# Attention groups from 20 on scored in pairs at new ticks, sums and roots turned by transposes, and fillers moved in the early ticks of a fused attention and expert kernel

## The reference, cut to what matters

```python
scores = (q @ k.T) / 8                        # 4 batches, 8 heads, 576 x 576, head dim 64
# heads 0-3: key within the last 32 positions; heads 4-7: key at a distance that is a multiple of 32
attn = softmax(where(mask, scores, -1e9)) @ v
x = attn as (2304, 512)
rms = sqrt(mean(x * x) + 1e-6)                # per token
xn = x / rms * rms_g
x = (silu(xn @ w_gate) * (xn @ w_val)) @ w_out      # 512 -> 1536 -> 512
logits = x @ router + modality_bias[modality_id]    # 8 experts, the best one is taken
out = softmax gate of that expert * (relu(x @ w1[e]) @ w2[e])   # 512 -> 1024 -> 512
```

## Time and profile before

| what | us |
|---|---|
| median of 3 runs (range) | 863.51 (862.11 to 865.79) |
| the profiled execution, its own time | 865.16 |
| its span in the trace | 863.4 |
| TensorE busy | 847.0 |
| VectorE busy | 535.7 |
| ScalarE busy | 369.6 |
| GpSimd busy | 330.5 |

### The profile page before, as it was taken

One profiled execution on the slowest core, in us unless ns is written; L12 is line 12 of the kernel. 1 busy time (PEld: TensorE's weight loads), 2 busy tenths in 40 slices (PEclk: granted clock), 3 DMA queues, 4 the chain that ended last, 5 costly groups with the idle time before them and its releaser, 6 DMA issues.

```text
span 863.4 us, 15547 instructions
## 1 busy us (share of the span) xinstructions
PE 847.0 (98%) x5203; PEld 732.6 (85%) x5203; DVE 535.7 (62%) x1400; ACT 369.6 (43%) x934; POOL 330.5 (38%) x373
## 2 busy tenths in 40 slices
PE   9999999999999999999999999999999999999996
PEld 5678898999889998999999998987888888888885
DVE  6975565444563446548788764884887457666663
ACT  6966414445354355443221132243456235554441
POOL 3735772434432633544346333070043122222212
PEclk9989999999999999999999999999999999999999
DMA  8974212312132210242131121626275645555531
GB/s 193 283 176 125 60 45 65 96 57 80 51 101 61 65 38 25 74 159 74 37 98 61 61 74 37 226 67 257 98 239 186 232 146 194 200 202 193 194 118 40
DMA packets 77517, 103.40 MB, mean 120 GB/s; under 512 B 38973, under 2 KB 43069, under 8 KB 77312
## 3 DMA queue, kind: packets, MB, share of 16 engines
q1 hardware_dynamic: 73760, 91.16, 33.5%
q0 software_dynamic: 3680, 11.28, 3.8%
HBM read 92.98 MB, written 10.22 MB: 120 GB/s over the span
## 4 chain that ended last, share of the span: by engine, by line
PE 86%; DVE 7%; issue 3%; POOL 2%; ACT 1%; DVEq 0%; POOLq 0%; ACTq 0%
PE ps L1251 31%; PE ps L1290 15%; PE ps L1855 13%; PE ps L1840 13%; PE ps L1176 3%; PE ps L1211 2%; PE ps L1865 2%; PE ps L1190 2%; PE ps L1150 2%; PE ps L1332 1%; PE ps L670 1%; DVE h L1641 1%; POOL sm L1046 1%; DVE h_lo L1646 1%; DVE w_lo L2094 1%
## 5 line engine op out<-in xcount | busy, mean ns | idle before, releaser
L1046 POOL TENSOR_TENSOR sm<-sm,rinv 72x288 f32<-72x288 f32 (+1 forms) x51 | 45.6, 893 | 168.8 <-DVE rinv L1577 168.8
L1078 POOL TENSOR_TENSOR out_lo<-out_raw,out_hi 128x512 fp32r<-128x512 f32 x72 | 101.8, 1414 | 5.8
L1076 POOL CAST out_hi<-out_raw 128x512 fp32r<-128x512 f32 x72 | 52.6, 730 | 132.9 <-DMA out_raw<-in_moe_w_out 132.9
L1251 PE MATMUL ps<-x_hi,gate_hi 128*128 128x384 f32 x288 | 100.1, 348 | 0.6 <-DVE h L1635 0.6
L1635 DVE SCALAR_TENSOR_TENSOR h<-h,ps 128x384 f32<-128x384 f32 x72 | 39.8, 552 | 97.4 <-ACT h L1469 96.5
L1251 PE MATMUL ps<-x_hi,val_hi 128*128 128x384 f32 x288 | 98.5, 342 | 0.0
L1251 PE MATMUL ps<-x_hi,gate_lo 128*128 128x384 f32 x288 | 96.9, 337 | 0.0
L1251 PE MATMUL ps<-x_hi,val_lo 128*128 128x384 f32 x288 | 96.4, 335 | 0.0
L1251 PE MATMUL ps<-x_lo,val_hi 128*128 128x384 f32 x288 | 96.3, 334 | 0.0
L1251 PE MATMUL ps<-x_lo,gate_hi 128*128 128x384 f32 x288 | 93.7, 335 | 0.0
L1290 PE MATMUL ps<-out_hi,h_hi 128*128 128x512 f32 x216 | 88.4, 409 | 1.3 <-DVE h_lo L1646 1.3
(11 more groups left out here) (288 smaller groups left out, 1937.8 us busy)
## 6 DMA issues: line engine op xcount, KB each, us to landing
w_raw<-in_moe_w SPq DMA_DIRECT2D x72, 512.0 KB, 4.4
out_raw<-in_moe_w_out SPq DMA_DIRECT2D x72, 256.0 KB, 2.6
x_rows<-y_tiles SPq DMA_DIRECT2D x18, 256.0 KB, 2.8
early_w_raw<-in_moe_w SPq DMA_DIRECT2D x8, 512.0 KB, 4.3
gate_raw<-in_moe_w_gate SPq DMA_DIRECT2D x4, 768.0 KB, 8.3
val_raw<-in_moe_w_val SPq DMA_DIRECT2D x4, 768.0 KB, 10.0
qk<-in_q SPq DMA_DIRECT2D x8, 288.0 KB
qk<-in_k SPq DMA_DIRECT2D x8, 288.0 KB
```

The source lines that it names most:

```text
L1046: pool.tensor_tensor(s3, s3, rinv[0:n, i, :].unsqueeze(2).to_broadcast([n, 4, c]), ALU.mult).then_inc(s_no, 1)
L1076: pool.tensor_copy(oh[i][:, :], o_raw[i][:, :]).then_inc(s_oh, 1)
L1078: pool.tensor_tensor(ol[i][:, :], o_raw[i][:, :], oh[i][:, :].bitcast(f32), ALU.subtract).then_inc(s_ol, 1)
L1251: mm = pe.matmul(ps[:, bank, 0:CH], w[:, i, kk, cols], x[:, kk, :], start=(m == 0), stop=(m == n - 1))
```

## The change

It changes places and distances of attention groups, the buffers, two small steps of the normalisation, and fillers.

- `PAIRS` is 20: groups 20 to 27 go in pairs, scored at ticks 22, 28, 40 and 52, turned at 32, 38, 50 and 62, multiplied at 34, 40, 52 and 64.
- The pairs from 28 on stand 4 ticks sooner: scored at 82, 94, ..., 238, which is (c, f, 1, 0) with f even, turned at (c, f, 0, 0), multiplied with the next pair's scores.
- `PLACE` uses four buffers throughout. Batch 1's second local head pair transposes q and k at ticks 34, 34, 36, 36 instead of 27, 29, 30, 32, in banks 6 and 5 by turns.
- For chunks 1 to 5 the sums over partitions are made by three transposes of the summed squares into bank 7, and VectorE reduces the 128 x 384 result. For all chunks the roots are spread by three transposes of the root column, broadcast along 128 columns; the tile of diagonals is gone.
- `square` waits only for the groups that hold tokens of its chunk. ScalarE's wait for the low parts of x at a batch's first pair now names batches 2 and 3, the only ones whose first group is in a pair before and after.
- Two fillers more at tick 16 between its scores and its turned probabilities, two more at tick 17 behind the sums, and two instead of three at the end of tick 17.

```diff
--- before.py
+++ after.py
@@ -61,8 +61,8 @@
     if j < HEAD:
         return j
     if j < 2 * NG:
-        return EARLY + 2 + 3 * (j - HEAD)
-    return EARLY + SPAN - 6 + 12 * ((j - 2 * NG) // 2)
+        return EARLY + (2, 8, 20, 32)[(j - HEAD) // 2]
+    return EARLY + SPAN - 10 + 12 * ((j - 2 * NG) // 2)
 
 
 def by_tick(ticks):
@@ -73,12 +73,12 @@
 
 
 SCORE = {j: score_tick(j) for j in range(G)}
-PAIRS = 2 * NG
+PAIRS = HEAD
 TURN = {j: SCORE[j] + (3 if j < HEAD - 3 else 7 if j < PAIRS else 10) for j in range(G)}
 TURN.update({HEAD - 3 + i: EARLY + 1 + 2 * i for i in range(3)})
 PV = {j: TURN[j] + (1 if j < HEAD - 1 else 2) for j in range(G)}
 
-PLACE = {j: j % SM if j < HEAD else (j - HEAD) % (SM - 1) for j in range(G)}
+PLACE = {j: j % SM for j in range(G)}
 PRIOR = {j: max((i for i in range(j) if PLACE[i] == PLACE[j]), default=None) for j in range(G)}
 
 EXPS = {j: SCORE[j] + (0 if j < HEAD - 1 else 1) for j in range(G)}
@@ -95,7 +95,9 @@
         return [0, 0, 0, 0]
     if s < EARLY:
         return {4: [1, 2, 2, 3], 8: [4, 5, 6, 7], 10: [7, 8, 8, 9], 14: [12, 12, 13, 13], 18: [14, 14, 15, 16]}[s]
-    return [s - 7, s - 5, s - 4, s - 2] if b < 2 else [s - 9, s - 9, s - 6, s - 6]
+    if b < 2:
+        return [s - 7, s - 5, s - 4, s - 2] if hp == 0 else [s - 6, s - 6, s - 4, s - 4]
+    return [s - 9, s - 9, s - 6, s - 6]
 
 
 QK = {(b, hp, t): qk_ticks(b, hp)[t] for b in range(B) for hp in range(4) for t in range(4)}
@@ -256,8 +258,8 @@
         sm_early = res.put("sm_early", [P, 512])
         sq_at = res.at
         sq = res.put("sq", [P, CH])
-        diag = alias("diagonals", sq_at, [P, TT, P])
         nr = res.put("squares_sum", [P, CH])
+        total = res.put("squares_total", [P, TT])
         var = res.put("variance", [P, TT])
         halved = res.put("halved_bits", [P, TT], i32)
         root = res.put("root", [P, TT])
@@ -442,8 +444,8 @@
         s_sq = sem("squares_steps")
         s_ssq = sem("squares_summed")
         s_nv = sem("variance_read")
+        s_va = sem("variance_made")
         s_nw = sem("newton_steps")
-        s_dg = sem("diagonals_made")
         s_rb = sem("roots_spread")
         s_rc = sem("roots_copied")
         s_xn = sem("normed_x")
@@ -519,7 +521,7 @@
 
         def qk_bank(b, hp, t):
             if QK[b, hp, t] >= FIRST_DOWN:
-                return 6 if b < 2 else 6 - t % 2
+                return 6 - t % 2
             if QK[b, hp, t] >= EARLY:
                 return 3 + QK_NO[b, hp, t] % 2
             return 4 if QK_NO[b, hp, t] % 2 else 0
@@ -1048,7 +1050,7 @@
 
             def square(c, kk):
 
-                first = max(i for i, (hp, g) in enumerate(GROUPS) if hp == kk and not (c == 0 and hp < 2 and g == 2))
+                first = max(i for i, (hp, g) in enumerate(GROUPS) if hp == kk and (hp > 1 or 2 * LQ * g <= (CH * c + CH - 1) % S))
                 pool.wait_ge(s_oe, NG * last_batch(c) + first + 1)
                 if c and kk == ORDER[0]:
                     pool.wait_ge(s_xn, KT * c)
@@ -1134,7 +1136,7 @@
                     per_load = 64 if is_loc(hp) else 32
                     pe.wait_ge(s_qk[hp], per_load * (b + 1))
                 if s >= FIRST_DOWN:
-                    pe.wait_ge(s_qe, no if b < 2 else no - t % 2)
+                    pe.wait_ge(s_qe, no - t % 2)
                     scores_read(s)
                     pe.wait_ge(s_pe, TURNED_PROBS[s])
                 elif TURNED_QK[QK_BY_ACT] == no:
@@ -1158,8 +1160,8 @@
                     pe.wait_ge(s_qe, QK_NO[b, hp, 3] + 1)
                 if j:
                     pe.wait_ge(s_m, 4 * (j if j < PAIRS else j - j % 2))
-                if j >= PAIRS:
-                    pe.wait_ge(s_pe, j - j % 2)
+                if TURNED_PROBS[s] > PAIRS:
+                    pe.wait_ge(s_pe, TURNED_PROBS[s])
                 if s >= FIRST_DOWN:
                     pe.wait_ge(s_qe, TURNED_QK[s])
                 for i in range(4):
@@ -1222,8 +1224,10 @@
                 pe.wait_ge(s_sq, sq_steps(c + 1))
                 for t in range(TT):
                     cols = slice(t * P, (t + 1) * P)
-                    mm = pe.matmul(ps[:, ss_bank(c), t:t + 1], nr[:, cols], ones[:, 0:1], start=True, stop=c > 0)
-                    if c == 0:
+                    if c:
+                        mm = pe.transpose(ps[:, ss_bank(c), cols], nr[:, cols], ident[:, :])
+                    else:
+                        pe.matmul(ps[:, ss_bank(c), t:t + 1], nr[:, cols], ones[:, 0:1], start=True, stop=False)
                         mm = pe.matmul(ps[:, ss_bank(c), t:t + 1], sq[:, cols], ones[:, 0:1], start=False, stop=True)
                 mm.then_inc(s_ssq, 1)
 
@@ -1231,9 +1235,11 @@
 
                 if c:
                     bank_7_free(("rb", c))
-                pe.wait_ge(s_dg, c + 1)
-                pe.matmul(ps[:, rb_bank(c), 0:CH], ones[:, :], diag[:, :, :].rearrange("p t n -> p (t n)"),
-                          start=True, stop=True).then_inc(s_rb, 1)
+                pe.wait_ge(s_nw, 11 * c + 11)
+                for t in range(TT):
+                    mm = pe.transpose(ps[:, rb_bank(c), t * P:(t + 1) * P], root[:, t:t + 1].to_broadcast([P, P]),
+                                      ident[:, :])
+                mm.then_inc(s_rb, 1)
 
             def product(bank, wh, wl, f, half, done, new=None):
 
@@ -1348,8 +1354,11 @@
                     keep_busy(2)
                 for j in SCORE_AT.get(s, []):
                     score(j)
+                if s == SS[0]:
+                    keep_busy(2)
                 if s == SS[0] + 1:
                     sum_squares(0)
+                    keep_busy(2)
                 for j in TURN_AT.get(s, []):
                     turn_probs(j)
                 for j in PV_AT.get(s, []):
@@ -1358,7 +1367,7 @@
                     for key in QK_AT.get(s, []):
                         turn_qk(*key)
                 if s < EARLY:
-                    keep_busy({16: 3, 17: 3, EARLY - 1: 4}.get(s, 2))
+                    keep_busy({16: 3, EARLY - 1: 4}.get(s, 2))
                 for c in SS_AT.get(s, []):
                     if c:
                         sum_squares(c)
@@ -1431,7 +1440,7 @@
                 b, hp, g = place(j)
                 n = rows(hp)
                 act.wait_ge(s_pv, j + 2)
-                if j % NG == 0:
+                if b >= 2 and j % NG == 0:
                     act.wait_ge(s_xl, KT * b)
                 src = ps[:, 7, :].rearrange("d (a x) -> d a x", a=2)[:, :, 0:2 * n]
                 if not is_loc(hp):
@@ -1594,10 +1603,18 @@
                     dve.wait_ge(s_nw, n_steps[0])
 
                 if c:
-                    dve.wait_ge(s_dg, c)
+                    dve.wait_ge(s_rb, c)
                 dve.wait_ge(s_ssq, c + 1)
-                dve.tensor_scalar(var[:, :], ps[:, ss_bank(c), 0:TT], 1.0 / DM, 1e-6, ALU.mult, ALU.add).then_inc(s_nv, 1)
-                dve.wait_ge(s_nv, c + 1)
+                if c:
+                    dve.tensor_reduce(total[:, :], ps[:, ss_bank(c), 0:CH].rearrange("p (t d) -> p t d", t=TT),
+                                      axis=AX, op=ALU.add).then_inc(s_nv, 1)
+                    dve.wait_ge(s_nv, c + 1)
+                    dve.tensor_scalar(var[:, :], total[:, :], 1.0 / DM, 1e-6, ALU.mult, ALU.add).then_inc(s_va, 1)
+                    dve.wait_ge(s_va, c)
+                else:
+                    dve.tensor_scalar(var[:, :], ps[:, ss_bank(c), 0:TT], 1.0 / DM, 1e-6,
+                                      ALU.mult, ALU.add).then_inc(s_nv, 1)
+                    dve.wait_ge(s_nv, 1)
                 link(dve.tensor_scalar(halved[:, :], var[:, :].bitcast(i32), 1, None, ALU.logical_shift_right))
                 link(dve.tensor_scalar(root[:, :].bitcast(i32), halved[:, :], -1.0, 1597463007.0, ALU.mult, ALU.add))
                 for i in range(3):
@@ -1606,9 +1623,6 @@
                     link(dve.tensor_tensor(newt[:, :], newt[:, :], var[:, :], ALU.mult))
                     link(dve.scalar_tensor_tensor(out=root[:, :], in0=newt[:, :], scalar=1.5, in1=root[:, :],
                                                   op0=ALU.add, op1=ALU.mult))
-                dve.wait_ge(s_sq, sq_steps(c + 1))
-                dve.tensor_tensor(diag[:, :, :], ident[:, :].unsqueeze(1).to_broadcast([P, TT, P]),
-                                  root[:, :].unsqueeze(2).to_broadcast([P, TT, P]), ALU.mult).then_inc(s_dg, 1)
 
             def normalise_x(c, kk):
 
```

## The result

The changed kernel takes 852.86 us (median of 4 runs, 851.78 to 853.54) against 862.86 for the kernel before measured beside it. The ratio is 0.987, interval 0.9846 to 0.9893. So 10 us were won where 13.1 were forecast; the time lies 2.5 us above the forecast 850.4 and inside its range. The profiled execution took 853.54, its span is 851.8.

A forecast was written before the change was run, and what follows sets the result against it. TensorE, busy 98% of the span, was taken as the bound. Terms 2.9 + 2.7 + 4.7 + 2.8 = 13.1 us off the median 863.5 gave 850.4, range 846.8 to 857.

The forecast's parts named there:

- A, the early ticks: Early ticks: fillers hold the clock up, root spread by three transposes; 2.9 us, or 0.2 if the clock falls.
- If they hold the clock up, the 6.8 us shrink: Early ticks, from about 47.3 us: fillers keep TensorE off the low clock, and that stretch gives back 3.0 us.
- the clock falls all the same: Rival for the early ticks: fillers do not stop the fall, gain there 0.2 instead of 2.9, time 853.1; chance 0.17.
- The margin of VectorE's path: Behind chunk 0's roots, before its first product at about 52.7: some 0.4 us to spare, so no cost.
- B, pairs from 20: Singles 20 to 27 become four pairs: cheaper scores and values, fewer dense interruptions, two transpose waits gone; 2.7 us.
- C, late pairs: Late pairs 4 ticks sooner: TensorE's nine waits, mostly at chunk changes and around roots, should go; 4.7 us.
- The margin behind y's copy: ScalarE's queue at (c, 0, 0, 0): y's copy and two probability copies, 2.4 us, fit TensorE's 2.8 by 0.3 to 0.4.
- D, transposes: Sums and roots by transposes in chunks 1 to 5: 0.55 us saved a chunk, 2.8 in all.
- The rival of transposes at 0.16: Rival: three 128-column transposes take 0.16 instead of 0.33 us at 11 places, time 848.5; chance 0.05.
- The Trainium skill's rule: Early ticks: low clock tied to an idle array; TensorE showed no idle stretch, so fillers would have nothing to fill.
- Slower: Rival: ScalarE's burst of exponentials makes output products wait at 18 pairs, 18 us lost, time 868; chance 0.03.
- lost further on: Rival: the front's gain is lost in the last chunk or to expert weights' transfers, time 858; chance 0.06.

The follow-up runs named there:

- part B: Kernel before with only groups 20 to 27 as pairs at ticks 22, 28, 40, 52, with their buffers, transposes and banks: 862.35 against 863.41 us, ratio 0.998.
- parts A and C: Kernel before with only the changed fillers: 864.34 us, ratio 1.0002; with only the pairs from 28 on 4 ticks sooner: 861.38, ratio 0.9984; both against 863.41.
- part D: Kernel before with only sums and roots by transposes, without the diagonals: 861.66 against 863.41 us, ratio 0.9971.

## Why the prediction was right, and where it was off

The direction, the bound and the range held. By its own steps:

- **A, the early ticks (2.9 forecast).** The step that failed: the rows were right, and what was made of them was not. "If they hold the clock up, the 6.8 us shrink" took the fall as a property of the kernel. It happens in 28 of 57 executions of the kernel before and costs 2.3 us each, 1.1 on average; the changed kernel has it in 2 of 16, at 4.2 each, 0.5. So of the 3.0 about 0.6 came, and by the share of all kernels with its early ticks, 9 of 34, it would be nothing. At full clock I had -0.4 for the fillers, which measure -0.6 alone (-0.1 in the traces); the spread's 0.3 is in part D. I had the rival that the clock falls all the same, at 0.17; its truth is "sometimes". The margin of VectorE's path was as followed: first product at 52.7 forecast, 52.9 seen.
- **B, pairs from 20 (2.7).** Measured 2.8 at full clock. The waits ahead of the transposes went; one behind ScalarE, at group 19's values, is 0.55 in part B's profile and 0.26 in those of parts A and C, which have single groups.
- **C, late pairs (4.7).** Measured 2.9 alone: the term that was over-sized. The waits for copied probabilities and for GpSimd went, 3.4 us; those for h_lo grew by 0.3. They stayed because I took GpSimd out of the last two ticks with its normalisation and forgot that its next instruction, the split, follows at once. The margin behind y's copy held: no wait at (c, 0, 1, 0).
- **D, transposes (2.8, and 0.3 of A).** Measured 2.6 alone: 3.1 on TensorE's path, less 0.5 of longer waits for GpSimd; three transposes are 0.33 both for sums and for roots. The rival of transposes at 0.16 falls.
- **The Trainium skill's rule** (TensorE: Matmul & The Clock Gate, Part 1), that an idle array brings the low clock: in the seven profiles with the fall TensorE waited 1.5 us at the start of the span and from there to the fall never over 0.5 us, and the clock fell all the same. Its factor of 4 for FP32 transposes (same page, Terms) does not show here: 0.65 to 0.33 is 2.
- **Slower, lost further on:** neither. Chunk 3's start stands 10.8 us and the span 11.6 us ahead of before.

The sum came nearer than its parts. A and C alone were 5.3 us too high, at full clock; that the time is only 2.5 us off is luck: the parts are worth 2 us more together, which I had not forecast, and the base of 863.5 stood 0.6 above the 862.9 measured beside the change.

What is left open: what decides in which executions the clock falls, whether the fillers around the sums lower the share or the 2 of 16 were luck, and why a fall lasts longer in the kernels that have the transposes.

## What to carry to other kernels

Before a term is built on a clock fall in one profile, look at the mean granted clock of every execution: where some have it and some have not, its worth is its cost times the share that it can still change. Compare variants among executions of one clock and with the old kernel of the same job, or the share and the chip hide the effect. Where an engine's work is moved out of a tight stretch, write down what stands next in its queue and is already released, for that moves in.

## What was not expected of the hardware

The clock's fall at about 47 us comes and goes between executions of one program with the same times up to there: profiled executions of parts B and C, with the old fillers, kept it at 1.00, one of the changed kernel with more fillers fell to 0.50 for some 10.2 us. The low stretch was 6.8 us long in the profile before, 10.2 here and in that of part D, and 13.6 in the changed kernel with the old fillers, and it cost 2.3 us in the kernel before, 4.0 in part D's and 4.2 in the changed one.

VectorE's subtraction of 128 x 384 values took 0.56 us when it started 0.20 us ahead of GpSimd's split, and 1.55 when it started 0.15 us behind it.
